# Entering the tile loop of a two-expert layer: register loads spread out, one tile's transposes moved, two chains of small operations interleaved

## The reference, cut to what matters

```
logits = x @ w_gate
noise_scale = np.log1p(np.exp(x @ w_noise))
noisy_logits = logits + noise_scale * noise
top2 = np.argpartition(-noisy_logits, 2, axis=1)[:, :2]
...
for e in range(E):
    for k in range(2):
        ...
        h = np.maximum(x[mask] @ w1[e], 0.0)
        out[mask] += top2_w[mask, k, None] * (h @ w2[e])
```

## Time and profile before

| | us |
|---|---|
| runs (3): lowest, median, highest | 1011.89, 1012.2, 1012.52 |
| the profiled execution's own time | 1011.48 |
| its span (first to last instruction) | 1009.6 |
| PE busy in it | 995.1 (99%) |
| DVE, ACT, POOL busy | 402.1, 430.0, 202.8 |

### The profile page before, as it was taken

One profiled execution on the slowest core, in us unless ns is written; L12 is line 12 of the kernel. 1 busy time (PEld: TensorE's weight loads), 2 busy tenths in 40 slices (PEclk: granted clock), 3 DMA queues, 4 the chain that ended last, 5 costly groups with the idle time before them and its releaser, 6 DMA issues.

```text
span 1009.6 us, 21781 instructions
## 1 busy us (share of the span) xinstructions
PE 995.1 (99%) x5892; PEld 856.8 (85%) x5893; DVE 402.1 (40%) x789; ACT 430.0 (43%) x736; POOL 202.8 (20%) x198
## 2 busy tenths in 40 slices
PE   8999999999999999999999999999999999999996
PEld 7889998998998998989778888888888888888885
DVE  3565642433433434436563222242366364222221
ACT  3347755554555455567522222232365453222221
POOL 4540000020010200200332222222222232222222
PEclk9999999999999999999999999999999999999999
DMA  8753360000000000053325221243276452211111
GB/s 269 260 161 136 125 219 1 1 32 1 1 31 0 0 31 0 29 192 125 84 56 207 63 73 59 66 160 118 89 244 241 135 177 67 69 53 53 53 48 45
DMA packets 47080, 95.27 MB, mean 94 GB/s; under 512 B 19245, under 2 KB 24749, under 8 KB 42928
## 3 DMA queue, kind: packets, MB, share of 16 engines
q1 hardware_dynamic: 24240, 66.23, 19.1%
q0 software_dynamic: 10992, 27.84, 8.5%
q10 hardware_dynamic: 11808, 0.68, 0.8%
HBM read 78.95 MB, written 20.37 MB: 98 GB/s over the span
## 4 chain that ended last, share of the span: by engine, by line
PE 95%; issue 1%; DMA 1%; DVE 1%; ACT 1%; ACTq 0%; POOL 0%; DVEq 0%; SPq 0%; POOLq 0%
PE bank L715 28%; PE bank L717 27%; PE bank L716 27%; PE bank L861 3%; PE bank L807 2%; PE bank L666 2%; PE bank L640 2%; PE bank L659 1%; PE bank L626 1%; PE bank L679 1%; PE bank L765 1%; DMA kdec<-c_k 1%; PE bank L772 0%; DMA prev<-out,meta_y 0%; DMA out<-ysb,meta_y 0%
## 5 line engine op out<-in xcount | busy, mean ns | idle before, releaser
L715 PE MATMUL bank<-ew,hT_hi 128*128 (+1 forms) x328 | 131.6, 401 | 1.7 <-DVE hT_lo L1476 1.7
L715 PE MATMUL bank<-ew,xgT_hi 128*128 (+1 forms) x328 | 131.8, 402 | 0.7 <-issue 0.7
L715 PE MATMUL bank<-xs_hi,mw 128*128 128x384 f32 x384 | 129.9, 338 | 0.0
L717 PE MATMUL bank<-xs_hi,mw 128*128 128x384 f32 x384 | 129.6, 337 | 0.0
L716 PE MATMUL bank<-xs_lo,mw 128*128 128x384 f32 x384 | 128.9, 336 | 0.0
L717 PE MATMUL bank<-ew,xgT_lo 128*128 (+1 forms) x328 | 128.3, 391 | 0.0
L717 PE MATMUL bank<-ew,hT_lo 128*128 (+1 forms) x328 | 128.3, 391 | 0.0
L716 PE MATMUL bank<-ew,hT_hi 128*128 (+1 forms) x328 | 127.9, 390 | 0.0
L716 PE MATMUL bank<-ew,xgT_hi 128*128 (+1 forms) x328 | 127.7, 389 | 0.0
L715 PE MATMUL bank<-mw,g_hi 128*128 128x512 f32 x288 | 114.6, 398 | 0.0
L717 PE MATMUL bank<-mw,g_lo 128*128 128x512 f32 x288 | 113.7, 395 | 0.0
(11 more groups left out here) (195 smaller groups left out, 1649.8 us busy)
## 6 DMA issues: line engine op xcount, KB each, us to landing
raw<-w_ex SPq DMA_DIRECT2D x32, 1024.0 KB, 4.8
stage<-w_ff SPq DMA_DIRECT2D x16, 512.0 KB, 3.3
out<-blank SPq DMA_DIRECT2D x3, 1536.0 KB, 11.3
x_rows<-x2sb SPq DMA_DIRECT2D x6, 768.0 KB, 3.6
kbuf<-kN SPq DMA_DIRECT2D x16, 256.0 KB, 3.3
vbuf<-vN SPq DMA_DIRECT2D x16, 256.0 KB, 4.4
qbuf<-qT SPq DMA_DIRECT2D x15, 256.0 KB, 3.8
xg<-x_rows,meta_x POOLq DMA_INDIRECT x43
```

Source lines behind the costliest of these rows:

```text
L715: pe.matmul(o, a_hi, b_hi, start=first, stop=False)
L717: return pe.matmul(o, a_lo, b_hi, start=False, stop=last)
```

## The change

Six edits. (1) PE: the seven register loads are taken apart: `pair` and tile 2's slot between the halves of `expert_in(2)`, tile 3's slot after the second half, tile 4's after four of the eight k-tiles of `expert_out(1)`. (2) PE: the transposes of tile 3 move to before the last k-tile of `expert_out(1)`. (3) DVE: tile 3's split stands before the output addition of tile 1, no longer behind it. (4) DVE, last chunk only: the operations of `gate_count` and `gate_weigh` alternate in one new function. (5) SP: tile 3's row number is loaded into its register before the wait for the records. (6) POOL: in `gather_x` the two waits change places.

```diff
-            sp.wait_ge(rec_sent, 16 * 2 * TJ * NCH)
             sp.wait_ge(tab_done, 1)
             alone(sp, got_x[1], 16)
-            load_meta(sp, meta_x, 1, 3, ld_mx[1])
+            row = entry(sp, T_ROW, 3, 0, LIST - P)
+            sp.wait_ge(rec_sent, 16 * 2 * TJ * NCH)
+            sp.dma_start(meta_x[:, 1, :], lists[bass.ds(row, P), :]).then_inc(ld_mx[1], 16)
...
             def gather_x(s, count, free, known=N):
+                alone(pool, xgT_made, free)
                 alone(pool, ld_mx[s], count * 16)
-                alone(pool, xgT_made, free)
...
+            def expert_out_part(g, e, par, tiles, h_hi=hT_hi, h_lo=hT_lo):
+                for k in tiles:
                     if k % 4 == 0:
                         pe.wait_ge(hT_lo_done, g * 2 + k // 4 + 1)
...
             hidden_transpose(1)
-            expert_in(2, 0, 0, 0)
-            expert_out(1, 0, 0)
+            pe.wait_ge(w_lo_done[0], 2)
+            pe.wait_ge(xgT_lo_done, 3)
+            pe.wait_ge(relu_done, 2)
+            expert_in_part(0, 0, 0, range(KT))
             pe.wait_ge(tab_done, 1)
             pair = entry(pe, T_PAIR, 0, PAIR_LOW, PAIR_HIGH)
-            early = [slot_of(g) for g in (2, 3, 4)]
+            early = [slot_of(2)]
+            expert_in_part(0, 0, 1, range(KT)).then_inc(m1_done, 1)
+            early.append(slot_of(3))
+            pe.wait_ge(w_lo_done[1], 2)
+            pe.wait_ge(y_done, 1)
+            expert_out_part(1, 0, 0, range(FT2 // 2))
+            early.append(slot_of(4))
+            expert_out_part(1, 0, 0, range(FT2 // 2, FT2 - 1))
             tile_transpose(3, 1, 2)
+            expert_out_part(1, 0, 0, range(FT2 - 1, FT2)).then_inc(m2_done, 1)
             step(1, 0, early[0], early[1])
...
+            def gate_count_and_weigh(c, done):
+
+                begun = c * GATE_STEPS + done[0]
+                iota = spread(small[:, 0:E], 1, [P, TJ, E])
+                for k in range(2):
+                    last = dve.tensor_tensor(oneh[:, k, :, :], iota,
+                                             spread(tixf[:, :, k], 2, [P, TJ, E]), ALU.is_equal)
+                last.then_inc(gate_step, 1)
+                dve.wait_ge(gap_exp, c + 1)
+                dve.tensor_scalar(wts[:, 1, :], gap[:, 1, :], 1.0, 1e-9, ALU.add, ALU.add).then_inc(gate_step, 1)
+                alone(dve, gate_step, begun + 1)
+                dve.tensor_tensor(both[:, TJ, :], oneh[:, 0, 0, :], oneh[:, 1, 0, :], ALU.add)
+                dve.tensor_tensor(both[:, 0:TJ, :], oneh[:, 0, :, :], oneh[:, 1, :, :], ALU.add).then_inc(gate_step, 1)
+                alone(dve, gate_step, begun + 2)
+                dve.reciprocal(wts[:, 0, :], wts[:, 1, :]).then_inc(gate_step, 1)
+                alone(dve, gate_step, begun + 3)
+                dve.tensor_tensor(both[:, TJ + 1, :], as32(both[:, TJ, :]), as32(both[:, 1, :]), ALU.add
+                                  ).then_inc(gate_step, 1)
+                alone(dve, gate_step, begun + 4)
+                dve.tensor_tensor(wts[:, 1, :], wts[:, 0, :], gap[:, 1, :], ALU.mult).then_inc(gate_step, 1)
+                alone(dve, gate_step, begun + 5)
+                dve.tensor_tensor(both[:, TJ + 2, :], as32(both[:, TJ + 1, :]), as32(both[:, 2, :]), ALU.add
+                                  ).then_inc(picked, 1)
...
-            gate_count(c, done)
-            gate_weigh(c, done)
+            gate_count_and_weigh(c, done)
...
+            split_tile(3, 1)
             add_output(0, 1, False)
-            split_tile(3, 1)
```

More of the change, by code:

```diff
@@ L874, in expert_out @@
                                  k == 0, k == FT2 - 1)
-                last.then_inc(m2_done, 1)
+                return last
+            def expert_out(g, e, par, h_hi=hT_hi, h_lo=hT_lo):
+                pe.wait_ge(w_lo_done[1], e * 2 + 2)
+                at_least(pe, y_done, g)
+                expert_out_part(g, e, par, range(FT2), h_hi, h_lo).then_inc(m2_done, 1)
             def step(i, s, this, after):
@@ L1504, in split_second @@
                                   ).then_inc(w_lo_done[p], 1)
+            def gate_count_and_weigh(c, done):
[20 more added lines that the diff above has]
+                                  ).then_inc(picked, 1)
+                dve.wait_ge(tok_done, c)
+                dve.wait_ge(rec_sent, c * (16 * 2 * TJ))
+                alone(dve, gate_step, begun + 6)
+                for k in range(2):
+                    dve.tensor_copy(rec[:, :, k, 1].bitcast(F32), wts[:, k, :])
+                    last = dve.tensor_copy(rec[:, :, k, 0], tok[:, :])
+                last.then_inc(gate_step, 1)
+                done[0] += 7
             split_begin(0)
```

## The result

| | before | changed kernel |
|---|---|---|
| median of 20 runs, us | 1011.92 | 1010.48 |
| lowest, highest | 1011.17, 1013.34 | 1009.61, 1011.57 |
| span of the profiled execution | 1009.6 | 1008.7 |

The ratio is 0.9987, 95% interval 0.9981 to 0.9993: 1.4 us faster, forecast 1.6. That is 0.14%, inside the 0.2% that the prediction called "same", on its faster side. A later set of 11 runs of the same kernel gave 1010.25 against 1011.71, ratio 0.9986 (0.9977 to 0.9994).

The account below looks back on a forecast made before the run. PE, busy 99% of the span, was taken to bound the kernel. A gain of 1.65 us at the way in less 0.05 for the picks gave 1.6, so 1012.2 becomes 1010.6 us; range 1009.8 to 1011.7.

Parts of the forecast that it names:

- same: Whole kernel: a difference within about 0.2%, 2.0 us, cannot be told from no change; chance 0.76.
- The sum at the way in: Before the loop: tile 3's first product on PE starts at 527.06 us instead of 528.71, 1.65 us earlier.
- Its two terms: PE before the loop: the register loads' halt of 0.94 us goes; tile 3's halt of 0.94 us shrinks to 0.25.
- the second term: PE before tile 3's first product: earlier transposes cut the 0.94 us halt to 0.25, supposing ACT and DVE are free.
- The loads at nothing: PE's seven register loads, spread in groups of at most 2.1 us, are hidden under 3.8 us of lead and cost nothing.
- The residual halt of 0.25: Before tile 3's first product: 0.25 us of PE's halt stays, as the ACT and DVE splits outlast PE's own work.
- more than forecast: Rival: tile 3's remaining 0.25 us halt and the picks' 0.14 us hole also go, 2.0 us gained, 1010.2; chance 0.17.
- The picks at 0.05 us: Last chunk's gate on DVE: weight operations fit between the chained additions, delaying PE's counting product by 0.05 us.
- the case in which each added operation costs its full length: Rival at the picks: three weight operations cost some 0.5 us in all, time 1011.1 us; chance 0.13.
- Tile 3's rows: Gather before tile 3's transposes: SP's edit and earlier slots move it forward something like 1 us, so rows are there.
- The shift of the rest: Loop and tail: everything after tile 3's first product merely shifts, as a tile period is PE work and the tail follows.
- Slower: Rival at tile 4's gather: SP's weight loads, about 1 us sooner, delay it; 1014.3 us at over 0.2% slower; chance 0.04.

Follow-up runs that it names:

- fed: Kernels with all edits bringing tile 3's rows forward (SP's, POOL's, the alternation); two k-tiles without them: 1011.14 us against 1011.71 for the kernel before.
- the meta load later: Tile 3's transposes two k-tiles before the end, all feeding edits, ScalarE's tile 4 meta load behind tile 3's split: 1012.54 us, kernel before 1011.52.
- two k-tiles: Changed kernel with tile 3's transposes one k-tile (0.68 us) earlier: 1009.35 us against 1011.95 for the kernel before; once more, 1010.18 against 1011.52.

## Why the prediction was right, point by point

- **The sum at the way in, 1.65 us: shown.** The first product of tile 3 is 1.65 us earlier against the mark in both traces of the changed kernel. Its two terms stand alone as 1.00 (worked out 0.94) and 0.69 (0.7). DVE's order, which the prediction named as what the second term supposes, is worth 0.73: all of that term.
- **The number: in part luck.** The forecast of 1010.6 stood on a median of 1012.2 from three runs; twenty gave 1011.92, 0.3 lower, and the gain was 1.4 and not 1.6, so two small errors of opposite sign left the time only 0.1 us off. The three runs were spread over 0.6 us, the twenty over 2.2, and half of 0.6 is 0.3 where the range took 0.4. With an interval from 0.7 to 1.9 us the times alone could not tell 1.6 from 1.0; the traces can.
- **The loads at nothing: shown**, with the condition on it: seven loads together make a halt of 1.20 us in the same place. The lead there was 3.2 us and not the 3.8 taken from the other place; three loads fit under either.
- **The residual halt of 0.25: shown** (0.25), and gone with one more k-tile. The rival "more than forecast" was wrong in this part.
- **The picks at 0.05 us: mis-sized by little, 0.00.** The counting product follows the product before by 0.95 us with and without the alternation. The added operations cost PE nothing: the reciprocal starts 0.10 us after a sum that lasts 0.18. The Trainium skill (VectorE: DVE Perf Modes, "The DRAIN you can't avoid") says that the next operation does not start until the pipe is empty, and that one which is not held starts earlier. The trace sides with the second; the case in which each added operation costs its full length, 0.5 us by the prediction's estimate, did not come.
- **Tile 3's rows: the step that was wrong in size.** "Something like 1 us in all" was short for the issue (1.1 to 1.8) and too much for the arrival: between nothing and 1.2 us earlier against the mark, in the seven fed traces. It cost nothing, as the rows were in 0.1 and 0.6 us ahead of the transposes in the two traces of the changed kernel. Its two parts were about right (SP's register load 0.5 to 0.7, measured 0.6 on average; the slots 0.6, measured 0.7); only their sum was put low. What it had not at all is the longer gather, which takes up to all of it back. That the move could go no further without the feed is right (a wait of 0.57 us at one more k-tile); at the changed kernel's own place the feed is worth 0.15 us.
- **The shift of the rest: not exact.** The time from the first product of tile 3 to the last hidden transposes was 466.17 in the profiled execution before, 466.97 and 466.64 in the two of the changed kernel, and 466.06 to 467.02 over thirteen traces, the one with the meta load later left out. It differs between two executions of the same kernel by 0.3 and has no trend with the edits that these runs could show; that the 0.8 us between the first two is chance and not a price of the change is likely by this, but not shown.
- **Slower: not seen.** Tile 4's gather was issued 1.1 us later than before, at 525.75, and its transposes did not wait. With all loads in one group and with the meta load later a halt did come before tile 2's output (0.58 and 2.47 us); in both ScalarE's meta load stands right ahead of the split that PE needed.

## What to carry to other kernels

In these kernels register loads on TensorE were free as long as their group (0.69 us a load) was shorter than the work already issued ahead of them, 3.2 to 3.8 us; count both in the trace and split the group at that length. A moved transpose pays only as far as the whole chain behind it follows, so look for what stands in its way in the queues of the engines that split it: here one addition in front would have taken all of it back. When effects of 0.1% are hunted, compare distances from a common mark inside the traces, since the runs' times scatter by as much. And when two parts of an edit seem to do nothing singly, take the way they act on apart step by step: a step that varies by 0.7 us hides a gain of 0.7 in one trace.

## What the runs showed of the hardware that was not expected

A tile of the loop takes one of two times, alike over many tiles, and changes at most once in a trace, near 768 us. These are two pairs of neighbouring hidden transposes from the kernel before, of different stretches of the same execution:

```profile
564.81 1.03 PE L861 MATMUL bank<-square,hid 128*128 128x128 f32 x8
577.11 1.03 PE L861 MATMUL bank<-square,hid 128*128 128x128 f32 x8
...
835.60 1.03 PE L861 MATMUL bank<-square,hid 128*128 128x128 f32 x8
847.85 1.03 PE L861 MATMUL bank<-square,hid 128*128 128x128 f32 x8
```

12.30 and 12.25 us, the same instructions of PE, with a granted clock of 1.00 in both stretches. Rounding aside the two are 12.29 and 12.25; over the last 17 tiles the kernel before took 208.30 us and the first trace of the changed one 208.98, which is 0.7 of the 0.8 us between their loops. The kernel before went from 12.29 to 12.25 at a halt of 0.22 us near 768 us; the first trace of the changed kernel stayed at 12.29 there, the second went to 12.25; two k-tiles entered the loop at 12.25 once and at 12.29 once. So it belongs to the execution. In most traces the change comes with a halt there, but in the loads in one group it came without one. The difference lies in the products right behind each group of transposes: the first nine take 2.16 us in the slow case and 2.14 in the fast one behind the hidden transposes, and 2.17 and 2.15 behind the tile's. What decides it is open.
